# Four tiles of one expert ahead of the last tokens' routing in a fused attention and mixture-of-experts kernel

## What is computed

```python
for t in range(S):                                  # q, k, v: 4 batches, 8 heads, 768 steps, 48 wide
    y[:, :, t] = q[:, :, t] @ state                 # a delta rule scan
    v_old = k_n[:, :, t] @ state
    state = state + beta * outer(k_n[:, :, t], v - v_old)
x = y as (3072 tokens, 384)
x = max(0.01 * h, h) @ w_out,   h = x @ w_in        # w_in 384 x 2048
do_compute = x @ w_skip > 0                         # tokens that the experts see
e_idx = argmax(x @ w_gate)                          # one of 8 experts
for e in range(8):
    y[e_idx == e] = prob * (relu(x @ w1[e]) @ w2[e])     # w1 384 x 1024, w2 1024 x 384
out[do_compute] = x + y
```

## Time and profile before

| | us |
|---|---|
| device time, median of 3 runs (lowest to highest) | 923.7 (921.95 to 925.36) |
| the profiled execution's own time | 924.88 |
| its span, first to last instruction | 923.1 |
| PE busy in the span | 783.5 (85%) |
| DVE, ACT, POOL busy | 649.7, 492.8, 415.3 |

### The profile page before, as it was taken

One profiled execution on the slowest core, in us unless ns is written; L12 is line 12 of the kernel. 1 busy time (PEld: TensorE's weight loads), 2 busy tenths in 40 slices (PEclk: granted clock), 3 DMA queues, 4 the chain that ended last, 5 costly groups with the idle time before them and its releaser, 6 DMA issues.

```text
span 923.1 us, 27938 instructions
## 1 busy us (share of the span) xinstructions
PE 783.5 (85%) x10858; PEld 632.4 (69%) x10859; DVE 649.7 (70%) x1304; ACT 492.8 (53%) x1100; POOL 415.3 (45%) x500
## 2 busy tenths in 40 slices
PE   0113588999999999999999999999956899999986
PEld 0113567787878777877777888887735687788864
DVE  5378886888878888788888888854667735533382
ACT  4435364767666666666666766554455424421261
POOL 4313261636263535444554525343314646544563
PEclk9975599999999999999999999999977999999998
DMA  8893765686787677767677675330736834511100
GB/s 241 128 222 61 123 117 104 132 134 141 124 153 134 113 142 125 143 125 146 125 147 126 123 140 108 65 58 19 242 102 220 293 113 148 200 51 51 40 19 16
DMA packets 355238, 115.73 MB, mean 125 GB/s; under 512 B 330338, under 2 KB 346772, under 8 KB 354752
## 3 DMA queue, kind: packets, MB, share of 16 engines
q1 hardware_dynamic: 349408, 100.40, 53.0%
q0 software_dynamic: 3232, 7.64, 2.4%
q10 hardware_dynamic: 2496, 6.29, 1.8%
HBM read 60.39 MB, written 20.46 MB: 88 GB/s over the span
## 4 chain that ended last, share of the span: by engine, by line
PE 39%; DVE 17%; DMA 12%; SPq 11%; issue 9%; ACT 7%; POOL 3%; DVEq 1%; POOLq 0%; ACTq 0%
PE b_acc L828 8%; PE b_h L689 8%; PE b_acc L702 8%; PE b_h L812 7%; PE b_ch L627 3%; DVE stage L1321 3%; SPq L467 3%; DVE inv L1251 2%; DMA operands<-operands 2%; DVE inv L1257 2%; SPq L479 2%; DMA natq<-x_dram,id_in 2%; DMA t_dram<-inv 2%; ACT operands L847 2%; DMA natq<-in_q_dram 1%
## 5 line engine op out<-in xcount | busy, mean ns | idle before, releaser
L1637 POOL TENSOR_TENSOR stage<-stage 128x256 f16<-128x256 f32 x192 | 142.8, 744 | 248.7 <-ACT stage L847 247.8
L689 PE MATMUL b_h<-stage,wt 128*128 128x256 f16 x1728 | 221.0, 273 | 5.7 <-DVE stage L1184 4.7
L702 PE MATMUL b_acc<-wt,stage 128*128 128x384 f16 x1152 | 219.3, 327 | 1.9 <-POOL stage L1637 0.9
L689 PEld LDWEIGHTS b_h<-stage,wt 128*128 128x128 f16 x1728 | 158.4, 98 | 26.1 <-DVE stage L1184 6.3
L702 PEld LDWEIGHTS b_acc<-wt,stage 128*128 128x128 f16 x1152 | 107.0, 98 | 56.6 <-POOL stage L1637 3.6
L847 ACT ACTIVATE stage<-stage 128x256 f16<-128x256 f32 x192 | 80.0, 417 | 104.0 <-DVE stage L1321 102.9
L1321 DVE SCALAR_TENSOR_TENSOR stage<-b_h,stage 128x256 f32<-128x256 f32 x192 | 80.7, 420 | 44.3 <-ACT stage L958 42.5
L828 PE MATMUL b_acc<-wt,operands 128*128 128x384 f16 x576 | 103.0, 329 | 7.3 <-DVE operands L1555 7.2
L812 PEld LDWEIGHTS b_h<-y,wt 128*128 128x128 f16 x1728 | 100.0, 99 | 8.0 <-issue 5.8
L812 PE MATMUL b_h<-y,wt 128*128 128x128 f16 x1728 | 102.5, 221 | 3.1 <-DVE y L1184 2.9
L1627 POOL TENSOR_TENSOR operands<-masked,operands 128x512 f16<-128x512 f32 x48 | 57.9, 1207 | 71.2 <-ACT operands L847 71.2
(11 more groups left out here) (180 smaller groups left out, 1239.7 us busy)
## 6 DMA issues: line engine op xcount, KB each, us to landing
operands<-in_moe_w_dram SPq DMA_DIRECT2D x16, 1536.0 KB, 7.7
a_sys<-a_dram SPq DMA_DIRECT2D x24, 256.0 KB, 4.1
kc<-operands SPq DMA_DIRECT2D x22, 256.0 KB, 4.4
natq<-in_q_dram SPq DMA_DIRECT2D x24, 192.0 KB, 4.1
raw_v<-in_v_dram SPq DMA_DIRECT2D x24, 192.0 KB, 3.9
stage<-y SPq DMA_DIRECT2D x96, 48.0 KB, 2.0
x_dram<-stage SPq DMA_DIRECT2D x24, 192.0 KB, 2.8
out_dram<-stage SPq DMA_DIRECT2D x24, 192.0 KB, 3.2
```

The costliest lines, as they stand in the source:

```text
L689: mm = pe.matmul(b_h[f % 2][:, 0:GT], wt[0][:, a, d * FF + f * P:d * FF + (f + 1) * P], xT[:, g % 2, b, d, :], start=(i == 0), stop=(i == ...
L702: mm = pe.matmul(b_acc[w][:, 0:DM], g16[:, f % 4, a, w * P:(w + 1) * P], wt[1][:, b, f * DM:(f + 1) * DM], start=(f == 0 and (a, b) == PAR ...
L1637: pool.tensor_tensor(g16[:, f % 4, LO, :], g32[:, f % 4, :], g16[:, f % 4, HI, :], ALU.subtract).then_inc(g_lo, 1)
```

## The change

After batch 0 (20 of 24 tiles of tokens) the expert with most tokens in it, the star, gets up to `FIRST` = 4 whole tiles of its own, made of its first tokens. They take tile numbers 0 to 3, the loop's tiles begin at 4, and the star's later tiles hold the rest. The four are written out between the work that routes the last tokens:

- `route_star`, `route_first`, `first_list`, `first_ids`: choose the star, take its first tokens out of the later list, and list them.
- SP stores zeros to the last two groups' rows (`x2_zeros`), loads expert 0 earlier (after `y_out(G - 1)`), then waits for `star_ready`, reads the star's number, and loads its weights into slot 1, ahead of `x2_out(G - 2)` and `probs_out(0)`. Expert 1 is loaded after `probs_out(2)`, once the star's quarters are split.
- Quarters 0 to 2 of the star's weights are split in turn G at f 0, 4 and 8 (each after the part of `w_out` that it overwrites was used), the fourth after it.
- POOL gathers tile 0's rows in turn G after f 2 and tile 1's after f 5; PE transposes tile 0 at f 6.
- Batch 0's routing comes 2 to 3 steps earlier, and its ranks go to `b_gr`. `seats` come three at a time.
- The last batch's routing, its list and expert 0's splits stand between the parts of tiles 0 to 3.

The core of the diff:

```diff
             def turn(g):
@@ SP
+                if g == G - 1:
+                    x2_zeros()
+                    first_weights()
...
+            def first_weights():
+                sp.wait_ge(z_done, 2 * G)
+                load_w1(0, 0)
+                load_w2(0, 0)
+                sp.wait_ge(star_ready, 1)
+                sp.wait_ge(s_done, 2 * G)
+                e = sp.value_load(star_n[0:1, 0:1], min_val=0, max_val=E - 1)
+                load_w1(e, 1)
+                load_w2(e, 1)
...
@@ PE
-                    if (g, f) in ((G - 1, 10), (G, 5)):
+                    if (g, f) in ((G - 1, 7), (G, 5)):
                         ranks(g - G + 1)
+                    if (g, f) == (G, 1):
+                        first_list()
+                    if (g, f) == (G, 6):
+                        transpose_x(0)
...
+            def first_tile(t):
+                pe.wait_ge(xg_ready, t + 1)
+                pe.wait_ge(e_lo, 1 + 2 * t)
...
+                expert_up(1, 0)
+                if t == 0:
+                    gate_x(G - 1, 0)
+                    gate_x(G - 1, 1)
+                expert_up(1, 1)
+                if t == 0:
+                    gate_s(G - 1, 0)
+                    gate_s(G - 1, 1)
+                    pe.wait_ge(ew_ready, 3)
+                pe.wait_ge(yo_ready, 1 + t)
+                expert_down(t, 1, 0)
...
+                transpose_x(t + 1)
+                expert_down(t, 1, 1).then_inc(ea_done, 1)
+                if t == 0:
+                    ranks(2)
+                if t == 1:
+                    full_list()
...
@@ ACT and DVE, turn G
+                    if g == G and f in (0, 4, 8):
+                        first_split_hi(f // 4)
...
+                    if g == G and f in (0, 4, 8):
+                        first_split_lo(f // 4)
...
@@ POOL
+                    if (g, f) == (G, 2):
+                        first_row()
+                    if (g, f) == (G, 5):
+                        copy_in(0)
+                        gather(1)
...
+            for t in range(FIRST):
+                if t == FIRST - 2:
+                    pool.wait_ge(list_ready, 1)
...
+                    pool.wait_ge(prob_stored, 3 * 64)
...
+                tile_next(t)
...
+                tile_back(t)
```

More of the change, by code:

```diff
@@ new lines, in expert_down @@
+            def expert_down(t, i, half):
+                pe.wait_ge(e_lo, 1 + 2 * t + half + 1)
+                for f in range(4):
+                    for a, b in PARTS:
+                        last = half == 1 and f == 3 and (a, b) == PARTS[2]
+                        w0 = W1C + (4 * half + f) * DM
+                        mm = pe.matmul(b_acc[0][:, 0:DM], e16[:, half, a, f * P:(f + 1) * P], wt[i][:, b, w0:w0 + DM],
+                                       start=(half == 0 and f == 0 and (a, b) == PARTS[0]), stop=last)
+                return mm
@@ L1149, in tile @@
                 tile_in(t + 1)
-            for q in range(3):
-                act.wait_ge(here_ready, q + 1)
-                copy(place[:, 8 * q:8 * q + 8, 1], here[:, 8 * q:8 * q + 8], row_id[:]).then_inc(row_ready, 1)
             act.wait_ge(tiles_ready, 1)
-            tile_in(0)
             with act.Fori(0, E // 2) as e2:
@@ L1536, in _ @@
                                   ALU.mult).then_inc(place_ready, 1)
-            dve.tensor_copy(tile_n[:, 0, :], row[:, 2])
-            dve.tensor_copy(tile_n[:, 1, :], row[:, 3])
-            dve.tensor_tensor(total_n[:], row[:, 3, E - 1:E], row[:, 2, E - 1:E], ALU.add).then_inc(tiles_ready, 1)
+            hidden_low(0, 0)
+            gate_x_low(G - 1, 0)
+            gate_x_low(G - 1, 1)
+            first_split_lo(3)
+            hidden_low(0, 1)
+            gate_s(G - 1, 0)
+            gate_s(G - 1, 1)
@@ new lines, in _ @@
+            dve.wait_ge(gate_ready, NT)
+            route_best(2)
+            route_hot(2)
+            tile_in(1)
+            route_prob(2)
+            tile_out(0)
+            route_rank(2)
+            link(dve.tensor_tensor(cmp_m[:], b_gr[:, NT * E:(NT + 1) * E].unsqueeze(2).to_broadcast([P, E, NT + 1]),
+                                   tri_m[:], ALU.is_gt))
+            link(dve.tensor_reduce(row[:, 1], cmp_m[:], AX.X, ALU.add))
+            link(dve.tensor_tensor(row[:, 1], row[:, 1], star_next, ALU.max))
@@ L1553, in hidden_low @@
-            def hidden_low(t, half):
-                dve.wait_ge(e_hi, 2 * t + half + 1)
-                dve.scalar_tensor_tensor(e16[:, half, LO, :], b_h[half][:], 0.0, e16[:, half, HI, :],
-                                         ALU.max, ALU.subtract).then_inc(e_lo, 1)
+            hidden_low(2, 1)
+            split_lo(0, 0, 2)
+            tile_in(3)
+            tile_out(2)
+            split_lo(0, 0, 3)
+            for t in range(3, FIRST):
+                hidden_low(t, 0)
+                hidden_low(t, 1)
+                tile_in(t + 1)
+                tile_out(t)
```

443 lines of the change are left out of this document (281 added, 162 removed).

## The result

| | before | changed |
|---|---|---|
| device time, median (15 runs each) | 925.16 | 920.04 |
| lowest to highest | 921.76 to 928.86 | 915.38 to 925.76 |
| ratio | | 0.994 (0.992 to 0.996) |
| profiled execution, own time | 924.88 | 921.86 |
| its span | 923.1 | 920.1 |

A forecast was written before the change was run, and what follows sets the result against it. PE was taken to bound the kernel outside a 22.7 us hole. Terms -33.0, +16.8, -2.7 and +8.0 sum to -10.9 us, giving 912.8 us from the median of 923.7; the range was 904 to 921.5.

The forecast's parts named there:

- turn G and the end of G - 1 (T to D): From turn G - 1's transposes to the last `down`'s end: added PE, DVE, ACT and POOL work costs +8.0 us, bounds 2.0 to 14.
- front (D to L): From the last `down`'s end to the loop's first tile: 39.5 us instead of 22.7, so +16.8.
- The hole, the star, the four tiles: PE's 22.7 us routing gap gets filled; expert 4 supplies four whole tiles, total stays 24, the end loses 33.0 us.
- Expert 0 to 2 behind it: The loop's first three tiles: about 30.5 us instead of 33.2, so -2.7, bounds 0 and -5.
- The star's block: Batch 0's DVE block: ten more linked steps delay `leaky` by 2.2 us, 1.0 is regained, so +1.2.
- Three quarters: Turn G: the star's splits at f 0, 4 and 8, ahead of `hidden` and `leaky`, cost +2.4 us.
- POOL's gathers: Turn G: two gather issues of 2.57 and 3.2 us, each in front of a `hidden_low`, cost +2.4.
- Star tiles at POOL's pace: Rival: tiles 0 to 3 go at 11.7 us each, front 46.8, +7.3, total 920; chance 0.11.
- Absorbing buffers: Rival: turn G costs 2 to 3 us instead of 8, the layout's waits shrink by 2, total 905 to 907; chance 0.12.
- Late rows: Rival: star's weights or probabilities land 8 to 10 us late, ACT or POOL blocks in turn G, total 921 to 923; chance 0.07.
- The low clock: Rival: pauses put tiles 0 to 3 at 1.2 GHz, +33 us, total 946; chance 0.04 together with missing whole tiles.
- The likeliest case: The forecast's own mechanism and sum for the whole kernel, 906 to 918 us; chance 0.66.

The follow-up runs named there:

- e3: The changed kernel with only expert 2's weight load held back until tile 4's rows are in; 916.6 us, ratio 0.990 to the kernel before.
- e5: The kernel before with only its first batch's routing two to three steps earlier, nothing of the star; 925.8 us, ratio 1.002.
- e1: The changed kernel with only `route_star` moved from step 8 to 9 of turn G - 1, behind one `leaky`; 915.7 us, ratio 0.988 to the kernel before.
- e4: The changed kernel with the star's quarters 0 to 2 split only 64 of 1536 columns wide; 913.6 us, ratio 0.990 to the kernel before.
- a1: The changed kernel run again without edits, as a level for other runs; 917.7 us, ratio 0.991 to the kernel before.
- f1: e7 with the star's quarters 0 to 2 split in halves of 768 columns; 908.7 us, ratio 0.985 to the kernel before.
- e2: The changed kernel with only the star's third quarter moved from step 8 to 9 of turn G; 916.6 us, ratio 0.990 to the kernel before.
- e6: The changed kernel with only tile 0's transposes and their split one step later in turn G; 916.8 us, ratio 0.992 to the kernel before.
- e7: The changed kernel with the edits of e1, e2, e3 and e6 together; 909.0 us, ratio 0.986 to the kernel before.
- a2: The changed kernel run once more without edits, on another chip; 915.9 us, ratio 0.993 to the kernel before.

## Why the prediction was right or wrong

| term | forecast | changed, by the ruler |
|---|---|---|
| four tiles off the end | -33.0 | -33.0 |
| turn G and the end of G - 1 (T to D) | +8.0 | +9.1 |
| front (D to L) | +16.8 | +15.9 |
| first three tiles and the rest, L to end | -2.7 | +1.8 |
| sum from T | -10.9 | -6.2 |
| ahead of T | 0 | +3.2 |

The last term is 191.2 less 189.4, which is 222.4 without the four tiles. T to L was forecast 24.8 longer and is 25.0 longer (25.2 and 25.0 in the repeats): nearly the whole miss lies behind L. The sum from T is -5.9 and -6.8 in the repeats, and its term behind L +1.9 and +1.3.

**The hole, the star, the four tiles: right.** There are 24 tiles again. From the fourth loop tile to the end (763.83 to 920.1) it takes 156.3 us; before, from 733.91, it took 189.2, 32.9 more.

**The step that failed: "Expert 0 to 2 behind it".** It gave -2.7, with bounds of 0 and -5; it was +1.8 (+1.9 and +1.3 in the repeats), outside its bounds each time. The reason that I wrote down for the gain, "expert 2's load starts earlier against its use", is what cost: the load now runs beside tile 2's scatter, which takes 8.1 instead of 3.1. With 8.25 us a tile, one `yout` and a DVE queue in order, that becomes a wait. e3, which takes only the overlap away, gives 31.2 for the three tiles, close to the 30.5 of the forecast, and -1.7 for the term. In the kernel before, the scatters at 713.32 and 724.63 took 6.4 and 6.5 beside loads and cost nothing, since its tiles came 10 to 12 us apart: each `tile_out` waited for POOL's copy (2.06 at 722.93) and none for a scatter. I had looked at whether each load was in time for its user, and not at whom it would slow down; the bound on the side of a loss was missing.

**Turn G: the sum nearly right by luck, its parts not.** Forecast against measured:
- `first_list` 1.5, measured 0.5 (667.26 to 667.77): its matmuls are 8 columns wide, and I had priced them by the list's 66. The list's row was slow besides: it ran at a granted clock of 0.50, and at the upper level 8 such matmuls take 0.41 (712.14) instead of 0.60.
- The star's block 1.2, measured about 4.3: a wait of 3.73, and `up` and `down` longer by 1.6 at the lower level of the clock (granted 0.50 from 648.97 to 650.87), less the 0.99 waited in the kernel before. The ten steps were priced rightly: 2.2 forecast, and they add 2.0 to the 1.76 of e5. What failed is the credit of 1.0, since the early place by itself costs 0.8 more (e5), and the clock, which the term left out. That PE "just bore" the block was the warning. e1 undoes 3.7 to 3.9 of it.
- Three quarters 2.4, measured 5.0 to 5.2 up to L and 4.1 up to D (e4 against a1). f1 didn't lower it by halves, which suggests, but doesn't show, that DVE and ACT have little room for the work itself in turn G; e2's place, behind the last `leaky`, is the one that helps.
- POOL's gathers 2.4, measured nothing by themselves: with the quarters thin, both waits for POOL go with all gathers in place. The issues took 1.13 and 1.03 in turn G, where I had used the 2.57 of the earlier trace rows. That one ran beside a quarter on DVE, which I had not looked for:

```profile
693.18 1.76 DVE L1184 SCALAR_TENSOR_TENSOR wt<-operands,wt 128x1536 f16<-128x1536 f32 x1 [0.70 <-POOLq L1741]
```

Two terms too low and two too high met at 9.1 for 8.0. The bounds (2 to 14) held.

**The front: right, by parts that cancel.** 38.6 for 39.5. The third list part waited 1.50 (forecast 0.8), tile 0's `up` lost 1.4 to the clock, and the other waits and the list's matmuls were smaller than laid out. The last batch's routing is covered as predicted; tile 4's transposes wait for no copy.

**The data was there.** The star's first weights were issued at 648.76, 2 us after the estimate, and ACT's first quarter at 665.73 waits for no DMA. The probabilities were issued at 658.38, and POOL's first gather, at 672.23, doesn't wait for them. Whether the rings are consumed in the order that *DMA: Bandwidth & Descriptors* in the Trainium skill (Queues, rings and completion order) states stays open, since nothing was close enough to tell.

**The port of DVE and POOL.** Beside a quarter of the loop's tiles (733.56 on DVE) POOL's copy takes 1.36 where 0.50 is usual, as the earlier trace rows had shown. The lock in *SBUF — State Buffer* of the Trainium skill (SBUF: two separate sides) lets one expect that, and the row agrees:

```profile
734.32 1.36 POOL L1885 COPY natk<-natq 128x384 f32<-128x384 f32 x1
```

In turn G no `hidden_low` met a quarter, and that term was rightly 0.

**The rivals.** Star tiles at POOL's pace: no, they came 10.8, 11.4, 8.2 and 8.3 apart, and no wait for a copy is among them. Absorbing buffers: no. Late rows: no. The low clock: not as a whole, but it is in three of the losses above (648.97, 690.13, 757.95), each time behind a wait of over 2 us. The likeliest case had the mechanism right up to the loop's start. Its own width (906 to 918) was too narrow: it counted on a gain behind that start and had no room for a new collision there.

**The signs.** One of the signs of being wrong appeared: PE waited 1.56 for a copy, that of tile 0's rows in turn G (679.35), which came late by the quarters (e4). The others did not: no quarter and no gather waited for data, `place` was waited for 1.50, and `down` in turn G waited 2.06 for POOL. The list had no sign for the tiles behind L, where the forecast failed. The last `down` ended at 690.3, 12.3 after 678.0 and outside the 5 to 11, by the 3.2 ahead of T.

**The two executions.** The 3.2 us ahead of T are no effect of the change: the repeats don't have them. They make the profiled pair (-3.0) a worse measure than the medians (-5.1, -7.7, -7.6).

## What to carry to other kernels

When a transfer moves earlier, list what it then runs beside, and above all the small transfers whose landing frees a buffer that is not doubled: their time to landing is the price, not the big one's. A stretch that the kernel "just bears" is at its limit: here what was added to it counted in full. So put new steps behind the next step that feeds a consumer, and not into the block. And compare two profiled executions from the last point at which they do the same, but check what that gives against the medians.

## What the runs showed of the hardware that I had not expected

- An indirect scatter of 128 rows of 384 fp32 took 8.1 us from issue to landing beside a weight load of 3 MB (8.2 and 8.5 in e4 and e6), and 3.1 without it (e7). At other places beside loads it took 6.4 to 6.8 (the kernel before), and 2.6 among the later tiles.
- Issuing an indirect gather took POOL 1.03 to 1.13 us, and 2.57 beside a quarter on DVE (693.36).
- Small matmuls are cheap when they are narrow: 20 of 8 columns in 0.51 us of PE's time; 8 of 66 columns took 0.41 at the upper level of the clock and 0.60 at the lower.
- After a wait of 2.06 us PE's next `up` took 3.58 and 3.67 us in two executions of the changed kernel (granted clock 0.57 and 0.55) and 2.17 in the third (a2, clock 1.00). There, behind the earlier wait of 3.74, three groups had run at the lower level (2.10, 2.13, 2.06; clock 0.50) instead of two. T to L was the same.
- Three executions of the changed kernel reach T between 634.2 and 639.4, 5 us apart, and from there on repeat within 0.9.
